# Attention and two MoE layers on one core: GpSimd fills half of a constant tile, rows are awaited per batch, and the sigmoid runs in other batches

## What is computed

```
for t in range(S):                       # B=2, H=8, S=768, D=40
    m_new  = max(f_gate[t] + m, i_gate[t])
    f_stab = exp(f_gate[t] + m - m_new);  i_stab = exp(i_gate[t] - m_new)
    C = f_stab * C + i_stab * outer(v[t], k[t])
    n = f_stab * n + i_stab * k[t]
    y[t] = sigmoid(o_gate[t]) * (C @ q[t]) / max(|n . q[t]|, 1)
x = leaky_relu(x @ w_in, 0.01) @ w_out                 # 1536 x 320 -> 2048 -> 320
P = exp(logits - max), 8 rounds of row and column normalisation, times N / E
out = sum over 8 experts of P[:, e] * (relu(x @ w1[e]) @ w2[e])
```

## Time and profile before

| | |
|---|---|
| time, median of 3 runs | 978.95 us (977.99 to 979.36) |
| the profiled execution: its time, its span | 980.03 us, 978.3 us |
| PE busy | 966.0 us, 99% of the span |
| DVE, ACT, POOL busy | 43%, 30%, 7% |
| mean granted clock of TensorE | 0.996 of full speed |

### The profile page before, as it was taken

How to read it: one execution, slowest core, us unless ns; L and a number is a source line. 1 busy time by engine, 2 the same in 40 slices (tenths; PEclk the granted TensorE clock), 3 DMA queues, 4 the chain that set the end, 5 groups by cost and what they waited for, 6 DMA issues and landing times.

```text
span 978.3 us, 14661 instructions
## 1 busy us (share of the span) xinstructions
PE 966.0 (99%) x5314; PEld 852.0 (87%) x5324; DVE 416.2 (43%) x821; ACT 296.7 (30%) x566; POOL 66.4 (7%) x120
## 2 busy tenths in 40 slices
PE   7999999999999999999999999999999999999998
PEld 4998888887788998889999899999888999989987
DVE  7677565545632552442333244223424422342222
ACT  5675344334522221221223122112312211321110
POOL 3364000000000331000000000000000000000000
PEclk9999999999999999999999999999999999999999
DMA  6962100300030030012003000300300030000000
GB/s 118 215 121 70 62 1 0 119 1 1 14 105 1 1 119 1 0 46 72 1 1 118 1 1 8 110 0 0 118 0 0 0 118 0 0 0 0 27 27 27
DMA packets 68190, 39.65 MB, mean 41 GB/s; under 512 B 52126, under 2 KB 64286, under 8 KB 68158
## 3 DMA queue, kind: packets, MB, share of 16 engines
q1 hardware_dynamic: 67950, 39.12, 15.3%
q10 hardware_dynamic: 208, 0.11, 0.0%
HBM read 37.03 MB, written 2.11 MB: 40 GB/s over the span
## 4 chain that ended last, share of the span: by engine, by line
PE 97%; ACT 2%; issue 1%; DVE 0%; SPq 0%; DMA 0%; DVEq 0%; POOL 0%; POOLq 0%; ACTq 0%
PE psA L1194 45%; PE psB L1232 12%; PE psB L1234 11%; PE psB L1233 11%; PE psB L1210 2%; PE psB L1212 2%; PE psB L1211 2%; PE psA L1090 2%; PE psB L1111 2%; PE psB L1217 1%; PE psB L1216 1%; PE psB L1138 1%; PE psA L1082 1%; PE psB L1101 1%; PE psA L1071 0%
## 5 line engine op out<-in xcount | busy, mean ns | idle before, releaser
L965 DVE SCALAR_TENSOR_TENSOR gl<-psA,gh 128x512 fp32r<-128x512 f32 x192 | 132.9, 692 | 335.6 <-ACT gh L716 335.5
L716 ACT ACTIVATE gh<-psA 128x512 fp32r<-128x512 f32 x192 | 114.9, 598 | 530.0 <-PE psA L1194 530.0
L1232 PE MATMUL psB<-w2s,gh 128*128 128x320 f32 x768 | 237.6, 309 | 0.0
L1233 PE MATMUL psB<-w2s,gh 128*128 128x320 f32 x768 | 237.3, 309 | 0.0
L1234 PE MATMUL psB<-w2s,gl 128*128 128x320 f32 x768 | 237.3, 309 | 0.0
L1194 PE MATMUL psA<-xh,w1h 128*128 (+1 forms) x480 | 189.9, 396 | 0.0
L1194 PE MATMUL psA<-xl,w1h 128*128 (+1 forms) x480 | 189.3, 394 | 0.0
L1194 PE MATMUL psA<-xh,w1l 128*128 (+1 forms) x480 | 188.6, 393 | 0.0
L1233 PEld LDWEIGHTS psB<-w2s,gh 128*128 128x128 f32 x768 | 144.3, 188 | 5.5
L1232 PEld LDWEIGHTS psB<-w2s,gh 128*128 128x128 f32 x768 | 144.2, 188 | 5.1
L1234 PEld LDWEIGHTS psB<-w2s,gl 128*128 128x128 f32 x768 | 144.4, 188 | 0.0
(11 more groups left out here) (159 smaller groups left out, 856.0 us busy)
## 6 DMA issues: line engine op xcount, KB each, us to landing
raw<-in_moe_w_dram SPq DMA_DIRECT2D x16, 640.0 KB, 8.3
raw<-in_moe_w_dram SPq DMA_DIRECT2D x8, 1024.0 KB, 5.5
raw<-in_moe_w_dram SPq DMA_DIRECT2D x16, 256.0 KB, 6.1
raw<-in_moe_w_out_dram SPq DMA_DIRECT2D x4, 640.0 KB, 7.5
qs<-in_q_dram SPq DMA_DIRECT2D x12, 160.0 KB, 3.2
ks<-in_k_dram SPq DMA_DIRECT2D x12, 160.0 KB, 3.6
vz<-in_v_dram SPq DMA_DIRECT2D x12, 160.0 KB, 3.6
og<-in_o_gate_dram SPq DMA_DIRECT2D x12, 160.0 KB, 3.8
```

The source lines that it names most:

```text
L716: act.activation(gh[:, f % RING, :], h_ps[:, f % HB, :], ACT.Relu).then_inc(ghi_ok, 1)
L965: dve.scalar_tensor_tensor(out=gl[:, f % RING, :], in0=h_ps[:, f % HB, :], scalar=0.0, in1=gh[:, f % RING, :].bitcast(F32), op0=ALU.max, o ...
L1232: pe.matmul(bank, gh[:, slot, cols], W2S[par][:, f, 0, :], start=first, stop=False)
L1233: pe.matmul(bank, gh[:, slot, cols], W2S[par][:, f, 1, :], start=False, stop=False)
```

## The change

Four things are done.

The constants of slot 1 for batch 1 are written by one GpSimd `tensor_tensor` of 128 x 1024 elements with two broadcast inputs, behind a wait on `parts_ok` (DVE's last write of `parts`), in place of eight DVE instructions behind `weigh(0, 0)`. `slot_ok` and `rows_in` become one semaphore for each batch, so that `exponents` of one batch waits only for its own two transfers.

The output gates of unit 2 are loaded behind the rows of chunk 1, and those of unit 3 move to the next group.

The sigmoid runs over units 0 to 2, 3 to 6 and 7 to 11 instead of 0 to 3, 4 to 7 and 8 to 11. The first is put behind the exponentials of unit 2, the other two between the copies of q and k of units 3 and 7 and the exponentials of the next unit.

Of the matmuls on zeros, the first run has 8 instead of 14, and the one ahead of `exponents(0, 0)` 9 instead of 4.

```diff
@@ sync
             load_v(1)
             load_qk(2)
-            load_gates_out(0, range(B, U_IT))
             sp.wait_ge(lhs_ok, 2)
-            sp.wait_ge(slot_ok, 1)
+            sp.wait_ge(slot_ok[0], 1)
+            sp.wait_ge(slot_ok[1], 1)
             sp.wait_ge(bounced, 16)
             chunk_rows(sp, 1)
+            load_gates_out(0, B, OG[1])
             load_v(2)
...
                     if n == U_IT:
-                        load_gates_out(1)
+                        load_gates_out(1, OG[1], OG[2])
                     if n == 2 * U_IT - 1:
-                        load_gates_out(2)
+                        load_gates_out(2, OG[2], OG[2] + 3)
+                    if n == 2 * U_IT:
+                        load_gates_out(2, OG[2] + 3, OG[3])
@@ gpsimd
             pool.wait_ge(blank, 1)
+            pool.wait_ge(parts_ok, 1)
+            pool.tensor_tensor(rhs[1][:, 1, :, :], head_rows[:].unsqueeze(2).to_broadcast([P, H, L]),
+                               at_row[:].unsqueeze(1).to_broadcast([P, H, L]), ALU.add).then_inc(slot_ok[1], 1)
             corner(0)
@@ scalar
             qk_copies(0, 1)
+            exponentials(0, 2)
             out_gates(0)
-            exponentials(0, 2)
             for n in range(2, NU):
                 i, j = n // U_IT, n % U_IT
-                act_unit(i, j)
+                qk_copies(i, j)
+                if n in OG[1:-1]:
+                    out_gates(OG.index(n))
+                    exponentials(i, j + 1)
+                high_parts(i, j - 2)
                 if n in PIECE_OF:
                     high_piece(0, 0, PIECE_OF[n])
-                if n < NU - 1:
+                if n not in OG[1:-1] and n < NU - 1:
                     exponentials(i, j + 1)
-                if n == U_IT:
-                    out_gates(1)
-                if n == 2 * U_IT:
-                    out_gates(2)
@@ vector
-            fill(1, 0)
+            fill(1, 0).then_inc(slot_ok[0], 1)
...
             weigh(0, 0)
-            fill(1, 1).then_inc(slot_ok, 1)
@@ tensor
-                    pe.wait_ge(rows_in[c % 2], ROWS * ((c + 1) // 2))
+                    pe.wait_ge(rows_in[c % 2][b], ROWS * ((c + 1) // 2))
...
-            warm(14)
+            warm(8)
             transposes(0, 0)
             warm(9)
             scores(0, 0)
-            warm(4)
+            warm(9)
             exponents(0, 0)
```

More of the change, by code:

```diff
@@ L211, in build @@
         copied_ok = sem("copied_ok")
-        slot_ok = sem("slot_ok")
+        slot_ok = [sem(f"slot_ok{b}") for b in range(B)]
         parts0_ok = sem("parts0_ok")
@@ L216, in build @@
         row0_in = [sem(f"row0_in{b}") for b in range(B)]
-        rows_in = [sem(f"rows_in{s}") for s in range(2)]
-        ROWS0, ROWS = (PARTS + 1) * 16, (B + B) * 16
+        rows_in = [[sem(f"rows_in{s}{b}") for b in range(B)] for s in range(2)]
+        ROWS0, ROWS = (PARTS + 1) * 16, 2 * 16
         blank = sem("blank")
@@ L242, in build @@
         qk_done = sem("qk_done")
-        og_in = [sem(f"og_in{i}") for i in range(NU // U_IT)]
+        OG = [0, 3, 7, NU]
+        og_in = [sem(f"og_in{i}") for i in range(len(OG) - 1)]
         sig_done = sem("sig_done")
@@ L307, in chunk_rows @@
             for b in range(B):
-                eng.dma_start(lhs[s][0:AR, b, :], parts_d[b, :, c, 0, :, :]).then_inc(rows_in[s], 16)
-                eng.dma_start(rhs[s][AR:M0, b, :, :], parts_d[b, :, c, 1, :, :].rearrange("h k t -> k h t")).then_inc(rows_in[s], 16)
+                eng.dma_start(lhs[s][0:AR, b, :], parts_d[b, :, c, 0, :, :]).then_inc(rows_in[s][b], 16)
+                eng.dma_start(rhs[s][AR:M0, b, :, :], parts_d[b, :, c, 1, :, :].rearrange("h k t -> k h t")).then_inc(rows_in[s][b], 16)
         def low_piece(eng, s, par, n):
@@ L363, in load_v, with load_gates_out @@
                 sp.dma_start(vz[j][:, :, 0:D], v[b, :, rows, :].rearrange("h s d -> s h d")).then_inc(v_in[j], 16)
-            def load_gates_out(i, units=range(U_IT)):
-                for j in units:
-                    n, c, b = unit(i, j)
+            def load_gates_out(i, first, end):
+                for n in range(first, end):
+                    c, b = n // B, n % B
                     sp.dma_start(og[:, n, :].rearrange("p (h d) -> p h d", d=D),
@@ L399, in _ @@
             load_qk(1)
-            load_gates_out(0, range(B))
+            load_gates_out(0, 0, B)
             sp.wait_ge(lhs_ok, 1)
@@ L554, in out_gates @@
             def out_gates(i):
-                act.wait_ge(og_in[i], U_IT * 16)
-                tile = og[:, i * U_IT:(i + 1) * U_IT, :]
+                act.wait_ge(og_in[i], (OG[i + 1] - OG[i]) * 16)
+                tile = og[:, OG[i]:OG[i + 1], :]
                 act.activation(tile, tile, ACT.Sigmoid).then_inc(sig_done, 1)
@@ L585, in qk_copies @@
                 last.then_inc(qk_done, 1)
-            def act_unit(i, j):
-                qk_copies(i, j)
-                high_parts(i, j - 2)
             def high_piece(s, par, n):
@@ L861, in finish_y @@
                 dve.wait_ge(fin_step, FIN * n + FIN)
-                dve.wait_ge(sig_done, i + 1 if j >= 0 else i)
+                dve.wait_ge(sig_done, sum(n >= first for first in OG[:-1]))
                 at_least(dve, e_done, n - 1)
```

## The result

The changed kernel takes **982.29 us**, median of 6 runs (981.82 to 984.0), against 979.08 of the kernel before on the same chip (977.65 to 979.99): a ratio of 1.0038, with an interval of 1.0025 to 1.0051. It is 3.2 us slower, where I had forecast 978.6. The profiled execution took 982.19 us with a span of 980.5; the span before was 978.3.

The account below looks back on a forecast made before the run. The prediction took PE to bound the kernel, for 97% of its chain. Gains of 0.6 (low clock, fill included) less 0.25 (later sigmoids) made 0.35, so 978.95 − 0.35 = 978.6 us; range 975.4 to 980.2 us, rivals included.

Parts of the forecast that it names:

- The fill moves to GpSimd: Early attention: POOL's fill stops a DVE fill; PE's 2.1 us transfer wait becomes 2.2 us for `gates_ok`, 0.1 us lost.
- first rival: At slot 1's fills, DVE and POOL don't stop each other, or POOL gives way: 3.4 us gained, 975.5 us; chance 0.25.
- The low clock: PE up to unit 3's exponents: low stretch unchanged (−0.1) or gone (+1.3); middle taken, +0.6 us gained.
- second rival: PE's clock falls earlier, by 17.3 instead of 20.9, slowing work up to `new_state` by 2.8 us: 982.1 us; chance 0.12.
- The sum 982.1: Time in us forecast by the second rival: 978.95 + 0.1 + 2.8 + 0.25.
- The two later sigmoids: Second and third sigmoid, ahead of the next unit's exponentials on ACT: intervals 7.6 and 7.9 us, 0.25 us lost for both.
- Loads, waits, zero matmuls: Moved gate loads, waits per batch and changed counts of matmuls on zeros: together 0 us.
- the cover of the second group's loads: Gate loads land at 33.3, their sigmoid begins at 36: 2.7 us spare, gone only in the first rival, costing perhaps 0.3.
- The sum against the median: Whole kernel: 0.35 us gained, taken from 978.95, the profiled execution's 980.03 less 1.08 to the runs' median: 978.6 us.

## Why the prediction was wrong

**The fill moves to GpSimd: right.** Forecast were a stopped fill of some 2 us (2.01, though the seventh and not the second), `dec_diag` near 15.8 (15.70), the exponents of unit 1 near 17.3 (16.98) and the wait for the rows gone (none left). POOL's instruction was priced at 2.1 and takes 1.90. That DVE and POOL exclude each other here is shown by the fills one behind the other, which take 1.65 and 1.90 us. The Trainium skill, page "SBUF — State Buffer", section "Who interferes with whom", describes such a lock for DVE's two-port modes; the trace agrees for the fill (2.01 us), and its two copies beside POOL's fill (0.36 and 0.26 us) show that not every DVE instruction falls under it. So the first rival (no lock, or POOL gives way until DVE's run is over) is refuted: POOL gave way for some 0.9 us only.

**The low clock: the step that failed.** I put its range from −0.1 ("the same low stretch") to +1.3 ("no low stretch") and took the middle, +0.6. Measured are −2.0. Both ends kept the stretch at its old place or took it away; that it could begin earlier I had only as a rival, with 0.12. But the reason for the rival stood in my own text: PE would stand for some 2 us ahead of 16.3 and 1.2 more behind, and before the clock had fallen in a wait of 2.1. With a wait of that length in a new place, a fall of the clock in that place was to be the forecast; it came in this profile and in that of the fill alone, and filling the wait took it away. What I held against it, a wait of 1.23 us up to 51.65 that left the clock at full, was half as long. Length isn't all of it, though: a wait of 2.85 us left the clock at full in the profile with the fills one behind the other, and no run here tells what sets such waits apart.

**The second rival: right in mechanism, wrong in its condition, lucky in its sum.** It said that the fall decides only if it lies before 17.3. It lay at 17.9, in the wait for ACT, and the price was still full, since of PE's work from the exponents of unit 1 to the end of `new_state` only these exponents' two matmuls lay before it. By the run with zero matmuls this work lost 2.84 us (6.06 less 3.22), for which I had 2.8. The stretch up to the exponents of unit 3 lost another 1.4 (8.40 less 7.01); before the change it was lost too (8.75), so it doesn't count between the kernels.

The sum 982.1 owes something to luck. Its terms, 0.1, 2.8 and 0.25, make 3.15 us, but the two profiles differ by 2.2, since the way from the exponents of unit 2 to those of unit 3 was 0.35 shorter than before, the exponents of unit 1 came 1.87 late instead of 2.2, and the sigmoids lost 0.05. And I had set the median 1.08 below the profiled execution, where the kernel after had both at the same place (982.29 and 982.19). The two errors cancel.

**The two later sigmoids: right in sum.** Forecast 7.6 and 7.9, measured 7.55 and 7.83, 0.05 us together against my 0.25.

**Loads, waits, zero matmuls: 0 holds only for this kernel.** The waits for gates did not appear after, and the zero matmuls gave nothing. But I had the cover of the second group's loads at 2.7 us, to be lost in the first rival alone, and its price, once gone, at 0.3. With the fill back on DVE the cover is gone and the price is 5: a wait of 2.0 on ACT, and behind it 10 us at the lower clock. With the fills one behind the other it is gone too, and the price is 1.7, as the clock stayed at full.

**The sum against the median.** The profiled execution before had a low stretch. Of the 64 runs of that kernel that stood beside the experiments, on three chips, 19 have a mean clock of 1.0 and take 977.7 to 978.1 us; the others, below 1.0, take 978.7 to 981.3. All six of the kernel after stand at 0.992 to 0.995. I reckoned from a single execution to a median of executions that differ by whether the clock falls; "no low stretch" was in part already in the median.

**Open.** Why the same kernel keeps its full clock in some runs and not in others isn't explained by anything that was run. Of the two waits in the kernel after, 2.38 and 1.21 us, the first decides: with zero matmuls in it the second one stayed and the clock was full, and with the fill alone the clock fell at 16.6, ahead of the second. What length of wait is too much was not tried, and since the clock fell at a wait of 2.38 us in one kernel and stayed at full through one of 2.85 in another, length alone doesn't answer it.

## What to carry to other kernels

A wait of TensorE of 2 us or more can let its clock fall; price it by the work that stands behind it at half speed, and not by its length alone. Here moving a wait of 2 us in front of busy work cost 3 us, and filling the same wait with matmuls on zeros gave 3.8 back. Before half of a job is given to GpSimd, look at what VectorE does at that very time: beside a run of short instructions one long one of GpSimd made `dec_diag` 2.09 us late, and behind that run it left `dec_diag` on time. And when a consumer is moved ahead, look for what feeds it: the gates' loads came too late for the moved sigmoid where SP began them at 28.1 us or later, and in time where it began them by 27.5.

## What had not been expected of the hardware

GpSimd did not always get in at once: in one kernel VectorE ran its fills up to the sixth beside it and GpSimd's instruction lasted 0.9 us longer, in the other it was in after the second one (it began at 12.37 us), and both times one fill was then stopped for GpSimd's whole remaining time (2.01 and 1.98 us). And the clock's fall is not the same in every execution: the kernel before shows a full clock in 19 of 64 runs, the kernel after in none of 6, and with eleven zero matmuls ahead of one wait the mean is 0.999 or 1.0 in 10 of 11.
